# Attention and a two-layer feed-forward part: inverse row sums spread by DMA through DRAM, remainder rows of q and k in one transpose, new orders on the engines

## The reference

```python
def rotate(x):                      # cos, sin: (576, 32), by position
    x1, x2 = x[..., :32], x[..., 32:]
    return concatenate([x1 * cos - x2 * sin, x1 * sin + x2 * cos], axis=-1)
scores = rotate(q) @ rotate(k).transpose(0, 1, 3, 2) / 8
attn = exp(scores - scores.max(axis=-1, keepdims=True))
attn = attn / (attn.sum(axis=-1, keepdims=True) + 1e-9)
a = attn @ v
x = a.transpose(0, 2, 1, 3).reshape(2304, 512)
h = x @ w_in
g = maximum(h, 0) + alpha * minimum(h, 0)
out = g @ w_out
```

## Time and profile before

| | |
|---|---|
| median of three runs | 701.14 us |
| the profiled execution's own time | 700.88 us |
| its span | 699.1 us |
| TensorE busy | 676.6 us, 97% |
| VectorE, ScalarE, GpSimd busy | 372.4, 314.2, 282.1 us |
| attention, up to the start of period 16 | 280.9 us |
| period 16 (the seam) | 280.9 to 296.4 us |

### The profile page before, as it was taken

How to read it: one execution, slowest core, us unless ns; L and a number is a source line. 1 busy time by engine, 2 the same in 40 slices (tenths; PEclk the granted TensorE clock), 3 DMA queues, 4 the chain that set the end, 5 groups by cost and what they waited for, 6 DMA issues and landing times.

```text
span 699.1 us, 12111 instructions
## 1 busy us (share of the span) xinstructions
PE 676.6 (97%) x4100; PEld 588.0 (84%) x4100; DVE 372.4 (53%) x681; ACT 314.2 (45%) x740; POOL 282.1 (40%) x258
## 2 busy tenths in 40 slices
PE   3899999999999999899999999999999999999996
PEld 3788888888888887698889999999999999999995
DVE  4688888888888878445642333233233323432231
ACT  2777777777777776333332222322322232223222
POOL 6655777777776504122222222222222222222221
PEclk9999999999999999999999999999999999999999
DMA  6897656666666642600001000000000010001001
GB/s 154 220 225 195 147 135 140 142 146 143 143 143 145 148 106 79 239 1 0 1 1 46 0 1 16 31 0 1 30 15 0 0 43 2 0 0 46 2 0 46
DMA packets 76619, 51.30 MB, mean 73 GB/s; under 512 B 61088, under 2 KB 61472, under 8 KB 76064
## 3 DMA queue, kind: packets, MB, share of 16 engines
q1 hardware_dynamic: 76576, 50.76, 28.9%
HBM read 22.95 MB, written 4.72 MB: 40 GB/s over the span
## 4 chain that ended last, share of the span: by engine, by line
PE 76%; issue 16%; POOL 2%; DVE 2%; DMA 1%; ACT 1%; SPq 1%; POOLq 0%; DVEq 0%; ACTq 0%
PE banks L620 19%; PE banks L647 19%; PE banks L547 14%; PE banks L505 12%; PE banks L566 10%; POOL g_lo L449 2%; PE banks L562 2%; DVE nmax L846 1%; DMA k_two<-k_hi 0%; DMA cos_sb<-in_cos 0%; DMA out<-stage 0%; DVE pt L895 0%; DVE k_lo L871 0%; ACT stage L807 0%; SPq L294 0%
## 5 line engine op out<-in xcount | busy, mean ns | idle before, releaser
L449 POOL TENSOR_TENSOR g_lo<-g,g_hi 128x384 fp32r<-128x384 f32 x96 | 99.3, 1035 | 312.2 <-ACT g_hi L795 306.1
L960 DVE TENSOR_SCALAR g<-banks,alpha_sb 128x384 f32<-128x384 f32 x96 | 59.3, 618 | 249.1 <-ACT pos L787 249.1
L620 PE MATMUL banks<-x_hi,w_in_lo 128*128 128x384 f32 x384 | 129.3, 337 | 0.0
L620 PE MATMUL banks<-x_hi,w_in_hi 128*128 128x384 f32 x384 | 129.2, 336 | 0.0
L620 PE MATMUL banks<-x_lo,w_in_hi 128*128 128x384 f32 x384 | 129.0, 336 | 0.0
L787 ACT ACTIVATE pos<-banks 128x384 f32<-128x384 f32 x96 | 47.1, 491 | 169.1 <-PE banks L620 169.1
L846 DVE TENSOR_REDUCE nmax<-banks 128x1 f32<-128x576 f32 x144 | 108.6, 755 | 22.8 <-PE banks L505 17.6
L647 PE MATMUL banks<-w_out_hi,g_hi 128*128 128x512 f32 x288 | 114.9, 399 | 1.6 <-POOL g_lo L449 1.4
L647 PE MATMUL banks<-w_out_hi,g_lo 128*128 128x512 f32 x288 | 112.9, 392 | 0.0
L647 PE MATMUL banks<-w_out_lo,g_hi 128*128 128x512 f32 x288 | 111.9, 389 | 0.0
L795 ACT ACTIVATE g_hi<-g 128x384 fp32r<-128x384 f32 x96 | 50.5, 526 | 119.7 <-DVE g L963 119.7
(11 more groups left out here) (83 smaller groups left out, 909.8 us busy)
## 6 DMA issues: line engine op xcount, KB each, us to landing
k_two<-k_hi SPq DMA_DIRECT2D x64, 160.0 KB, 2.9
out<-stage SPq DMA_DIRECT2D x18, 256.0 KB, 2.0
raw_q<-in_q SPq DMA_DIRECT2D x32, 128.0 KB, 2.8
raw_k<-in_k SPq DMA_DIRECT2D x32, 128.0 KB, 2.4
q_two<-q_hi SPq DMA_DIRECT2D x32, 128.0 KB, 2.3
q_two<-q_lo SPq DMA_DIRECT2D x32, 128.0 KB, 2.3
q_own<-q_hi SPq DMA_DIRECT2D x32, 128.0 KB, 2.4
raw_v<-in_v SPq DMA_DIRECT2D x32, 128.0 KB, 2.3
```

Source lines behind the costliest of these rows:

```text
L449: nc.gpsimd.tensor_tensor(g_lo[f % 2][:, :], g[f % 2][:, :], g_hi[f % 2][:, :].bitcast(F32), ALU.subtract).then_inc(g_lo_done, 1)
L620: mm = nc.tensor.matmul(h_ps[f % 2], w[:, j, cols], xx[:, j, :], start=(step == 0), stop=(step == 3 * CT - 1))
L960: nc.vector.tensor_scalar(g[f % 2][:, :], h_ps[f % 2], 0.0, alpha_sb[:, f:f + 1], ALU.min, ALU.mult).then_inc(neg_done, 1)
```

## The change

- Sums: `SUM_COLS` puts the remainder tile's sums into column 8 and the others into 0 to 7. One transpose of the 128 x 9 inverse gives nine rows of 128; VectorE copies them to `inv_rows_sb`; SyncE writes them to a DRAM tensor `inv_rows` of 2 x 576 (`put_inverse`, two DMAs) and, when these have landed, reads it back with each row repeated over 64 partitions into `inv_sb` (`get_inverse`, one DMA). The wide copy, the four transposes and the copies of U_INV and of the remainder go.
- Remainder of q and k: both lie in slot 4 of `raw_q` (partitions 0 to 63 and 64 to 127), are rotated together and turned by one transpose (U_REMS, in front of U_K). `raw_k` and `rot_k` have four slots instead of five. q's load has four DMAs, k's two; the cos and sin tables are loaded in two parts each.
- Orders: TensorE, ScalarE and VectorE have new lists; who copies which bank changes too (all of U_PA on ScalarE, U_KREM on VectorE, U_QREM on ScalarE).
- Seam: in period 15 the high part of x is made by ScalarE (`high_x`) and VectorE makes only the low part. In period 16 the second product with v has its own bank and waits for no normalise; hidden block 1 stands behind it.

```diff
-U_KQREM, U_QREM = 0, 1
-U_KREM = 2
-U_PB = (3, 4, 5, 6)
-U_Q, U_K, U_MIXED = 7, 8, 9
-U_INV = 10
+U_QREM, U_KQREM, U_INV = 0, 1, 2
+U_KREM = 4
+U_PB = (3, 7, 5, 6)
+U_Q, U_REMS, U_K = 8, 9, 10
 U_PA = (11, 12, 13, 14)
+SUM_COLS = (8, 0, 1, 2, 3, 4, 5, 6, 7)
...
+            return banks[:, 6 if h and not has_now(p) else 7, 0:HALF]
...
-                sp.dma_start(raw[0:REM, QT, :].rearrange("p (h d) -> p h d", h=2),
-                             src[bass.ds(p * 2, 2), QT * P:S, :].rearrange("h p d -> p h d")).then_inc(landed, 16)
+                if side == 0:
+                    for h, rems in enumerate((q_h, k_h)):
+                        sp.dma_start(raw_q[h * REM:(h + 1) * REM, QT, :].rearrange("p (h d) -> p h d", h=2),
+                                     rems[bass.ds(p * 2, 2), QT * P:S, :].rearrange("h p d -> p h d")).then_inc(q_in, 16)
...
+            def table(dst, src, landed):
+                sp.dma_start(dst[:, 0:QT, :], src[:, 0:QT, :]).then_inc(landed, 16)
+                sp.dma_start(dst[:, QT, :], src[0:REM, QT, :].unsqueeze(0).to_broadcast([2, REM, D])).then_inc(landed, 16)
+            def put_inverse(p):
+                sp.wait_ge(evac[U_INV % T_BANKS], evac_count(p, U_INV))
+                sp.dma_start(inv_rows[:, 0:QT * P].rearrange("h (i c) -> h i c", i=QT),
+                             inv_rows_sb[0:2 * QT, :]).then_inc(inv_put, 16)
+                sp.dma_start(inv_rows[:, QT * P:S], inv_rows_sb[2 * QT:TILES, :]).then_inc(inv_put, 16)
+            def get_inverse(p):
+                sp.wait_ge(inv_put, p * 32)
+                sp.dma_start(inv_sb[:, :], inv_rows.unsqueeze(1).to_broadcast([2, D, S])).then_inc(inv_in, 16)
...
                     load_v(b, t)
+                    put_inverse(p)
                     if has_pair(p + 2):
                         load(p + 2, 1)
+                    get_inverse(p)
...
+                if f == 4:
+                    put_inverse(PERIODS)
+                    get_inverse(PERIODS)
                 sp.dma_start(w_out_raw[:, f:f + 2, :],
...
# TensorE, period
-                turn(p, t, U_KQREM)
                 turn(p, t, U_QREM)
                 score(p, t, REM_TILE)
+                turn(p, t, U_KQREM)
+                turn(p, t, U_INV)
+                score(p, t, A_TILES[0])
                 if not has_now(p):
                     hidden(0, 0, 0)
-                turn(p, t, U_KREM)
-                score(p, t, A_TILES[0])
                 turn(p, t, U_PB[0])
-                turn(p, t, U_PB[1])
+                turn(p, t, U_KREM)
                 turn(p, t, U_PB[2])
                 score(p, t, A_TILES[1])
                 turn(p, t, U_PB[3])
+                turn(p, t, U_PB[1])
                 turn(p, t, U_Q)
                 score(p, t, A_TILES[2])
+                turn(p, t, U_REMS)
                 turn(p, t, U_K)
-                turn(p, t, U_MIXED)
                 score(p, t, A_TILES[3])
-                if not has_now(p):
-                    hidden(0, 0, 1)
                 pv(p, par, 0)
                 score(p, t, B_TILES[0])
-                turn(p, t, U_INV)
-                score(p, t, B_TILES[1])
                 turn(p, t, U_PA[0])
+                score(p, t, B_TILES[1])
                 turn(p, t, U_PA[1])
                 turn(p, t, U_PA[2])
-                score(p, t, B_TILES[2])
                 turn(p, t, U_PA[3])
+                score(p, t, B_TILES[2])
                 score(p, t, B_TILES[3])
                 pv(p, par, 1)
+                if not has_now(p):
+                    hidden(0, 0, 1)
...
+            def high_x(j):
+                act.wait_ge(x_done, 2 * (j + 1))
+                nc.scalar.activation(x_hi[0][:, j, :], x[:, j, 0:CHUNK], ACT.Copy).then_inc(x_high, 1)
```

More of the change, by code:

```diff
@@ L482, in score @@
                 if n == 0:
-                    for u in (*OF_NEXT, U_MIXED):
+                    for u in OF_NEXT:
                         pe.wait_ge(evac[u % T_BANKS], evac_count(p - 1, u))
@@ L528, in turn @@
                 elif u == U_INV:
-                    pe.wait_ge(wide_done, p)
-                    blocks = [inv_wide[:, i, :] for i in range(QT)]
+                    pe.wait_ge(inv_done, p)
+                    blocks = [inv[:, (t - 1) % 2, :]]
                 elif u == U_Q:
@@ L537, in turn @@
                 else:
[L538 to L544, removed]
+                    turned_in(p, 0)
+                    blocks = [rot_q[:, QT, :]]
+                rows = TILES if u == U_INV else P
                 for i, block_in in enumerate(blocks):
-                    i = 2 if at else i
-                    mm = nc.tensor.transpose(bank[:, i * P:(i + 1) * P], block_in, ident[:, :])
+                    mm = nc.tensor.transpose(bank[0:rows, i * P:(i + 1) * P], block_in, ident[:, :])
                 mm.then_inc(turned, 1)
@@ L559, in pv @@
                         pe.wait_ge(evac[u % T_BANKS], evac_count(p, u))
-                if not (isinstance(n, int) and n == 0):
+                if not (isinstance(n, int) and n == 0) and not (h and not has_now(p)):
                     pe.wait_ge(x_done, n)
@@ L740, in flat @@
                     jobs = [(pt[:, pt_slot(t % 2, 0, U_PA.index(u)), 0:QT * P], bank)]
-                else:
-                    jobs = [(inv_sb[:, 0:QT * P], bank)]
+                elif u == U_QREM:
+                    par = (t - 1) % 2
+                    jobs = [(pt[:, 0:3 * QT, QT * P:S].rearrange("p (h j) s -> p j h s", h=3)
+                             [:, :, par:3:2 - par, :], bank.rearrange("p (j h s) -> p j h s", j=QT, h=2))]
                 for dst, src in jobs:
@@ L849, in lo @@
             def lo(p, u, t):
-                if not exists_now(p, u):
+                if not has_next(p):
                     return
-                if has_next(p):
-                    dve.wait_ge(hi_done, hi_count(p, u))
-                else:
-                    dve.wait_ge(turned, unit_count(p, u))
+                dve.wait_ge(hi_done, hi_count(p, u))
                 bank = t_ps[u % T_BANKS]
@@ L874, in lo @@
                                                              op0=ALU.mult, op1=ALU.subtract)
-                if u == U_MIXED and has_prev(p):
-                    for r in HEADS:
-                        ins = nc.vector.tensor_copy(inv_sb[r, QT * P:S], bank[r, 2 * P:3 * P][:, r])
                 ins.then_inc(evac[u % T_BANKS], 1)
```

217 lines of the change are left out of this document (108 added, 109 removed).

## The result

| | before | after |
|---|---|---|
| median of four runs | 701.03 us (700.89 to 701.91) | 748.72 us (746.58 to 749.50) |
| ratio, 95% interval | | 1.0673 [1.0649, 1.0696] |
| span of the profiled execution | 699.1 us | 747.7 us |
| TensorE busy | 676.6 us | 690.8 us |

The change makes the kernel 47.7 us slower. 695.6 was forecast. The page of after, against the earlier trace rows: the header, part 1, the clock in 40 slices, the chain by engine, and two groups of part 6 (DMA issues; the last number of such a row is the median landing in us, which the page doesn't have for the read).

What follows compares the result with a forecast made beforehand. TensorE was taken to bound the kernel. From 700.88 us: + 3.75 by period 5, - 5.45 in ten middle periods, - 1.86 in period 15, - 1.96 in the seam, giving 695.4, or 695.6 as median; range 690.5 to 700.5.

Steps and rivals of the forecast that it cites:

- the landing of the inverse's read: SyncE's get in a middle period: issued at 6.6, landed by 9.6 to 10, used at 11.86, so the round trip is hidden.
- Rival B: DRAM round trip holds the stacks in every period: landing over 3.5 exceeds 16.07; at 4.6, 706.2 us; chance 0.08.
- the dispute on HBM under load: Landing of the inverse's put in periods 1 to 3: 2.2 us when quiet, 4 if loaded, adding some 4 us.
- late at period 5, by the first value product: Later start and SyncE's longer rounds in periods 1 to 3 make the new kernel 3.75 us late at period 5.
- a middle period, undisturbed: Middle periods, walked through the new queues: TensorE bounds them at 16.07 us, five transposes (0.545) less than before.
- rival A: SyncE's queue clears in periods 1 to 3, so only the start costs, + 1.4: 691.6 us; chance 0.26.
- rival C: ScalarE and VectorE's handshake binds: B4's slack of 0.14 is overrun, each of 14 periods loses 0.3, 699.9 us; chance 0.10.
- a slack of 0.4 to 0.5: Middle period: the last stack of q lands at 17.2, the next period's score A1 is due at 17.68.
- if rows of k_two appear as releaser after period 5: Sign that the prediction is wrong: TensorE's waits are released by k_two after period 5; no size given.
- Seam: Between period 15 and the first output block: 13.55 us instead of 15.51, with work 12.7 and 0.9 left; gain 1.96.
- Period 15: Last full period, half the splitting of x moved to ScalarE: 15.8 us instead of 17.66, with 0.7 of stalls; gain 1.86.
- If that cover fails ... 17.2: Period 15: if the splitting isn't hidden on ScalarE either, all 2.1 of stalls stay and it takes 17.2, + 1.4.

Runs made afterwards that it cites:

- E1: The changed kernel with the inverse read back by two DMAs, one for each head, instead of one: 701.29 us, ratio 0.9999 to the kernel before.
- E9: E1 with VectorE making q_lo in front of the fourth maximum (A4) instead of behind it: 697.24 us, ratio 0.9940 to the kernel before.
- E10: E9 with ScalarE's small copy of the remainder's columns also moved behind B2's exp, as in E5: 697.36 us, ratio 0.9940.
- E5: E1 with ScalarE's small copy of the remainder's columns moved from between the exps of B1 and B2 to behind B2's: 701.40 us, ratio 1.0001.
- E12: E10 with the cos and sin tables loaded by one DMA each instead of in two parts: 696.23 us, ratio 0.9924 to the kernel before.
- E14: E9 without write and reads of the inverse, inv_sb set to 1 once (not the reference): 698.10 us, ratio 0.9959.
- E15: E12 with the first chunk of x split by VectorE alone, high_x taken from ScalarE: 697.16 us, ratio 0.9949 to the kernel before.
- E4: The changed kernel with the inverse's read replaced by one plain read of 128 different rows of w_in (not the reference): 700.72 us, one run.
- E2: The changed kernel, its read's shape kept but taking 2 x 64 different rows of w_in (not the reference): 747.68 us, one run.
- E8: E1 without write and reads of the inverse, inv_sb all ones (not the reference): 700.58 us, ratio 0.9994 to the kernel before.

## Why the prediction was wrong

**The failed step** is the landing of the inverse's read: "get issued 6.6, landed by 9.6 to 10 (I take the 160 KB stack's 2.9; bounds 2.2 and 4.3), used at 11.86. The round trip itself is hidden in a middle period". Value and bounds came from DMAs of another shape, and the size was the only thing compared. It took 8.6 to 10.7 us at its ten places in the chain, median 10.1. Issued at 6.6 it would land at about 16.7, 4.8 after it is wanted; the longest wait of TensorE was 5.1. More followed, which the prediction put at nothing. TensorE stood still, and its clock fell to the lower level (4.04 for 2.09). And k_two landed late, most likely because the stacks share two engines with the read, which isn't shown for single engines. Its landings between 140 and 200 us, in after and in E1:

```profile
DMA to landing us min/median/max: 2.7/3.5/7.7
```

```profile
DMA to landing us min/median/max: 2.4/2.9/3.8
```

Where k_two is late, so is the next period's A1. How the 47 us divide among wait, clock and late stacks was not separated by a run: a kernel in which the long read lands in a tile that nobody waits for wasn't tried.

Rival B had the sign and the place (the DRAM round trip holds the period), but another mechanism, a slow write and loaded queues. The write landed in 1.6 to 2.0 us in E1's periods 1 and 2:

```profile
40.34 1.63 DMA inv_rows<-inv_rows_sb
...
56.25 1.98 DMA inv_rows<-inv_rows_sb
```

"The put lands in under 3 us" was right, and the dispute on HBM under load was about a term that did no harm: what the loaded figure would add isn't there. The write has an outermost dimension of 2 as well, with 4 KB in all: with so few bytes this shape cost nothing here.

**What the other steps were worth** is read from E1, where the read is as the prediction assumed. Its 701.3 is 5.7 above the forecast; in the profiled executions it is 7.1 at the first output block (297.99 us against 296.42 - 5.5).

| step | forecast, us | E1, us |
|---|---|---|
| late at period 5, by the first value product | 3.75 | 3.55 (107.42 against 103.87) |
| of it, start | 1.4 | 3.2 |
| of it, periods 1 to 3 | 52.5 | 50.1 |
| a middle period, undisturbed | 16.07 | 16.27 |
| ten middle periods | - 5.45 | - 0.3 |
| period 15 and seam | - 3.8 | - 1.6 |

- *Start and periods 1 to 3.* The sum is right, its parts are not, so the sum is luck. In E1's chain q_lo behind the fourth maximum and the issues behind it (25.73 to 32.62) hold period 0 as well, which the step left out; what that costs isn't fixed (E9 has 1.4 less, E10 nothing). And SyncE's queue cleared as rival A has it, so that distances of 17.06, 16.29 and 16.75 stand where 16.4, 17.6 and 18.5 were forecast.
- *Middle, 0.2 of each.* The five transposes are gone. B3 and B4 take 1.23 instead of 1.06. By E5 the small copy isn't why. The walk had B2's score ready 11.13 into the period; counted in the same way (from the first value product at 206.46, which the walk has at 6.89) its last matmul ends at 11.32 in E1. B2's exp then starts at 12.17 instead of 12.01 and B4's score at 13.06 instead of 12.97, the slack of 0.14 being used up. From a stand this score takes 0.64 to the value product, where the walk had 0.53, so that the product starts at 13.70 instead of 13.50. That is the whole 0.2. It is rival C's mechanism, with 0.2 of a period where it had 0.3, read from one timeline and tested by a run only as far as the small copy.
- *Middle, 3.5 us in six periods.* The walk gave k_two a slack of 0.4 to 0.5 and this was spent. In E1's period 13 the chain is

```profile
239.76 0.76 DVE nmax L891
240.52 0.61 DVE q_lo L913
241.15 0.50 SPq L299
...
243.62 2.08 SPq L300
...
248.31 3.10 DMA k_two<-k_hi
...
251.54 0.76 PE banks L536 x4
```

  An issue of 2.08 instead of 0.60 takes 1.5, more than the slack. The prediction named the sign of it, "if rows of k_two appear as releaser after period 5", and priced it at nothing. E9 prices q_lo's place at 4 us of the median, period 0 included. Why single issues stretch to 2.08 stays open.
- *Seam.* 14.75 instead of 13.55 (283.24 to 297.99), and 14.62 in E12. The work is 12.7 as forecast. The stalls were priced at 0.9 and are 2.1: 1.27 in front of the first transpose, where `normalise`, the remainder's sum and the reciprocal stand one behind the other on the path, and 0.82 at a bank's copy (289.29 to 290.11). The first of them:

```profile
283.26 0.46 DVE x L955
283.71 0.42 DVE rsum L940
...
284.15 0.23 DVE inv L944
284.38 0.14 issue
284.51 0.27 PE banks L573
```

- *Period 15.* 15.8 forecast, 16.08 in E12 (262.46 to 278.54), where k_two is in time. What is left of the stalls in that trace stands at ScalarE's copy and exp (266.88 to 268.33), not at x; in E14's it stands at x_lo, beside GpSimd's split. The late slab, which the prediction put at nothing, keeps the two apart. "If that cover fails ... 17.2" is too dear for E15's trace, in which VectorE makes both parts and 0.5 is lost.

With the read in two and q_lo in front, the kernel takes 696.2 (E12), 0.6 above the forecast. That is no proof of its steps: in E12 the middle period is 16.24 at best, the seam 1.1 longer than forecast, and the first three periods are shorter than forecast.

## What to carry to other kernels

Compare a new DMA with a row of the trace by its outermost dimension first and by its bytes second: the same 288 KB took 10.1 us with 2 outermost and 3.1 with 128. When an instruction is moved behind another, follow everything that waits for it to its end; a slack of 0.4 us behind ten issues and a landing is none. And a run that leaves work out also moves what stood behind it: E14 paid back in x_lo part of what it may have saved.

## What the runs showed of the hardware

- A read of 288 KB with an outermost dimension of 2 ran on 2 of 16 engines (share 0.13), and the DMAs beside it landed later: k_two's median over the kernel is 3.4 us, in E1 2.9.
- Reading one DRAM row 64 times costs little at most: 3.1 us for each 144 KB (E1), 3.1 for 288 KB of different rows (E4); with 2 outermost 10.1 against 9.5 (medians, after and E2).
- After TensorE had waited for 3.2 us its granted clock was 0.50 in the stretch behind (134.8 to 141.0); in stretches of full work it was 1.00 (107.4 to 108.6).
- VectorE's x_lo took 0.5 to 0.56 us without GpSimd's split of w_in beside it, and mostly 1.1 to 1.3 with it (E8, E14, E15; single ones 0.57 and 0.82).
- The write and the reads in GpSimd's queue instead of SyncE's, with a small operation in front of the write and one in front of the reads: 713.4 us instead of 701.3.
